# TensorE reads the present tile's slot and piece count at the top of the round instead of between y's transpositions and the second product

## The reference

```
# attention: y[b,h,t] = r_t (state + u k_t v_t); state = w_t * state + k_t v_t
x  = attention output as 3072 rows of 384
# first expert layer (float32)
expert_idx = argmax(normalised x @ normalised expert_emb.T / tau)
out[mask]  = gate_w[mask] * (relu(x[mask] @ w1[e]) @ w2[e])        # w1: 384x1024, w2: 1024x384
# second expert layer, on the rows of the first
e_idx = argmax(x @ w_gate)
out[mask] = gate_w[mask] * sigmoid(x @ w_output_gate)[e] * (relu(x[mask] @ w1[e]) @ w2[e])
```

## Time and profile before

| | |
|---|---|
| median of 3 runs | 810.31 us |
| the profiled execution | 813.64 us, its span from first to last instruction 811.9 us |
| granted TensorE clock, mean | 0.964 |
| PE busy | 727.1 us, 90% of the span |
| PEld (weight loads) busy | 638.3 us, 79% |
| DVE, ACT, POOL busy | 62%, 48%, 20% |

### The profile page before, as it was taken

The page is one execution under the profiler, slowest core; times in us unless marked ns, Lnnn a source line. Parts: engine busy times, 40 slices in busy tenths (PEclk is TensorE's granted clock), DMA queues, the critical chain, the costliest instruction groups (busy, mean ns, idle before and its releaser), DMA issues.

```text
span 811.9 us, 21320 instructions
## 1 busy us (share of the span) xinstructions
PE 727.1 (90%) x5494; PEld 638.3 (79%) x5495; DVE 503.7 (62%) x1363; ACT 390.8 (48%) x760; POOL 160.3 (20%) x202
## 2 busy tenths in 40 slices
PE   2898898980899999999999998499999999999994
PEld 2687687760688988888888887379999999999993
DVE  8899899986466674746675675544635444436621
ACT  4565777781355463535464464144534444425521
POOL 5354565553000000000000000001000000010000
PEclk9999999996799999999999999689999999999998
DMA  5655588635543351423352433233505152416110
GB/s 130 148 148 151 156 251 238 176 99 188 185 157 116 117 175 37 135 91 109 117 173 91 141 116 117 91 101 132 202 29 194 49 182 78 157 39 194 39 33 26
DMA packets 50267, 103.73 MB, mean 128 GB/s; under 512 B 7921, under 2 KB 29904, under 8 KB 50224
## 3 DMA queue, kind: packets, MB, share of 16 engines
q1 hardware_dynamic: 29536, 67.18, 26.9%
q10 hardware_dynamic: 15568, 21.76, 9.8%
q0 software_dynamic: 5120, 14.26, 4.8%
HBM read 85.73 MB, written 19.01 MB: 129 GB/s over the span
## 4 chain that ended last, share of the span: by engine, by line
PE 69%; DVE 8%; issue 8%; ACT 5%; DMA 4%; ACTq 2%; SPq 2%; POOL 1%; DVEq 0%; POOLq 0%
PE bank L1303 18%; PE bank L1329 17%; PE bank L1337 10%; PE bank L1308 9%; PE bank L1318 5%; DMA rk<-rk_in 3%; PE bank L1270 2%; PE bank L1292 2%; ACT wall L559 2%; DVE SF L765 2%; DVE Q L756 2%; PE bank L1124 1%; ACTq L246 1%; PE bank L1263 1%; POOL rkp L393 1%
## 5 line engine op out<-in xcount | busy, mean ns | idle before, releaser
L1303 PE MATMUL bank<-wall,xT_hi 128*128 (+1 forms) x660 | 180.1, 409 | 3.3 <-ACT xT_hi L651 3.3
L1329 PE MATMUL bank<-wall,hT_hi 128*128 x880 | 167.2, 341 | 0.8 <-ACT hT_hi L660 0.5
L1329 PEld LDWEIGHTS bank<-wall,hT_hi 128*128 128x128 f32 x880 | 154.6, 189 | 8.1 <-issue 5.5
L869 DVE TENSOR_TENSOR wall<-raw,wall 128x1024 f32 (+1 forms) x96 | 112.0, 1221 | 61.9 <-ACT wall L559 58.6
L1303 PEld LDWEIGHTS bank<-wall,xT_hi 128*128 128x128 f32 x660 | 119.7, 192 | 24.0 <-issue 4.0
L655 ACT ACTIVATE hs<-bank 128x512 f32<-128x512 f32 x110 | 65.1, 592 | 110.6 <-PE bank L1308 103.5
L559 ACT ACTIVATE wall<-raw 128x1024 f32 (+1 forms) x96 | 95.1, 1050 | 42.0 <-issue 42.0
L1308 PE MATMUL bank<-wall,xT_lo 128*128 (+1 forms) x330 | 94.5, 394 | 0.0
L660 ACT ACTIVATE hT_hi<-bank 128x512 fp32r<-128x512 f32 x110 | 59.8, 596 | 68.6 <-PE bank L1318 68.6
L1337 PE MATMUL bank<-wall,hT_lo 128*128 x440 | 91.0, 348 | 0.0
L1030 DVE TENSOR_TENSOR xT_lo<-bank,xT_hi 128x384 fp32r<-128x384 f32 x57 | 31.8, 558 | 87.9 <-ACT xT_hi L651 87.9
(11 more groups left out here) (194 smaller groups left out, 953.7 us busy)
## 6 DMA issues: line engine op xcount, KB each, us to landing
raw<-wall_in SPq DMA_DIRECT2D x96, 512.0 KB, 3.8
xin<-sorted ACTq DMA_DIRECT2D x59, 194.0 KB
rk<-rk_in SPq DMA_DIRECT2D x46, 192.0 KB
v_in<-v_src ACTq DMA_DIRECT2D x24, 192.0 KB
vT<-vT_in ACTq DMA_DIRECT2D x48, 96.0 KB
wb<-w_in SPq DMA_DIRECT2D x46, 96.0 KB
sorted<-padrow SPq DMA_DIRECT2D x16, 194.0 KB, 2.1
sorted<-yrow,slot POOLq DMA_INDIRECT x28, 2.6
```

What stands on the lines that cost most here:

```text
L869: v.tensor_tensor(w_lo[:, slot, cols], raw[:, q], w_hi[:, slot, cols].bitcast(F32), ALU.subtract).then_inc(w_split, 1)
L1303: pe.matmul(bank[n][:, :], xT_hi[:, k, :], w[:, bass.ds(slot, 1), cols].rearrange("p o n -> p (o n)"), start=(k == 0 and w is w_hi), stop= ...
L1329: pe.matmul(bank[2][:, 0:DM], hT_hi[:, j, :], w[:, bass.ds(slot, 1), W2 + j * DM:W2 + (j + 1) * DM].rearrange("p o n -> p (o n)"), start=( ...
```

## The change

The one line that loads the present tile's slot and piece count is moved up, behind the load of the next tile's.

```diff
@@ -1349,11 +1349,11 @@
                 with pe.Fori(0, last) as p:
                     slot, pieces = weights(p + 1)
+                    old_slot, old_pieces = weights(p)
                     transpose_h(p)
                     first_product(p + 1, 0, slot, pieces)
                     if m == 0:
                         transpose_y(p + 1)
-                    old_slot, old_pieces = weights(p)
                     second_product_hi(p, old_slot, old_pieces)
                     if m == 0:
                         logits_y(p + 1)
```

## The result

| | before | after |
|---|---|---|
| median of the runs | 810.71 us (6 runs, 808.7 to 811.85) | 851.67 us (6 runs, 849.94 to 854.34) |
| ratio | | 1.0508, 95% interval 1.0488 to 1.0528 |
| span of the profiled execution | 811.9 us | 852.6 us |
| granted clock, mean | 0.964 | 0.964 |

The kernel is 5% slower. It was forecast at 852.9 us, within 842 to 861.

What follows compares the result with a forecast made beforehand. TensorE (PE) was taken to bound both loops, with sequencer time free only while it is ahead. 25.5 + 9.6 - 2.0 + 9.5 = 42.6 us on a median of 810.31 gave 852.9 us, range 842 to 861.

Steps and rivals of the forecast that it cites:

- Cost of `weights`: Both loops: one `weights` call takes TensorE's sequencer 1.5 us, with bounds of 1.03 and 1.77 us.
- Slack in m=0: Top of m=0's rounds: sequencer's slack 0.43 us after rounds without splits, 0 after splits; VectorE's choice of expert sets it.
- Sum of m=0: Loop of m=0: 25.5 us at 17 tops without slack, plus 9.6 at nine others, less 2.0 in the middle.
- Middle: m=0, ahead of L1329: the 0.2 us wait goes, worth 2.0 us over 10 rounds without splits.
- Slack in m=1: Top of m=1's rounds: slack 1.15 us against 1.5 us added, costing 9.5 us over 27 rounds.
- C: Both loops: the sequencer reaches the top earlier by what the middle saves; 2.0 us faster, 808.3 us; chance 0.04.
- E: Both loops: the loads move but are done beside PE's work anyway; time within 0.2%; chance 0.03.
- Rival D: Loop of m=0: the clock falls to 0.96 as well, adding 5.6 us, time 858.5 us; chance 0.07.

Runs made afterwards that it cites:

- mid_early: The kernel before with the middle pair of loads moved one step earlier, ahead of `transpose_y`; 809.55 us, ratio 0.9975.
- carry: The kernel before with the present tile's two numbers copied in registers instead of loaded a second time; 808.98 us, ratio 0.9974.
- extra_top: The kernel before with an unused pair of value loads added at the top of each round, middle pair kept; 852.61 us, ratio 1.0489.
- only_m1: The kernel before with the read moved to the top in the loop of m=1 alone; 817.84 us, ratio 1.0072.
- extra_late: The kernel before with an unused pair of value loads added ahead of `ranks_y`, middle pair kept; 812.33 us, ratio 1.0017.

## Why the prediction was right, point by point

- **Cost of `weights`, 1.5 us.** Right. The wait is 1.57 to 1.70 us in the rounds after splits, 1.64 on the mean; 0.08 of it stood there before, and 0.04 comes back in the transpositions (below).
- **Slack in m=0 and its place.** Right. Waits of about 1.1 us after rounds without splits (1.5 - 0.43 = 1.07) and 1.6 after the others. The branch still follows VectorE's choice, by 0.10 to 0.14 us in all 26 rounds both before and after, and not the sequencer's saved time; in one round of the kernel after, L993 and the branch:

```profile
323.79 0.29 DVE L993 TENSOR_SCALAR oha<-iota,r 128x8 bf16<-128x8 f32 x1
```

```profile
L1350 PEldq ALU_OP  x1: 32/32/32, 324.2 to 324.2; - x1
```

- **Sum of m=0, forecast 33.1 us.** Measured 34.0: the first top comes 1.47 us later (within the trace, 3.95 us behind the value load of L1349 where it came 2.42); the round behind that entry is 1.50 longer; seven with the first pieces split 1.66 each; eight with the last split 1.51; ten without splits 0.74 on the mean (nine 0.86, and the last 0.36 shorter, since the transpositions behind the loop have no added pair ahead of them and the middle's wait is gone). The seven are 0.15 over the term of 1.5. The prediction had ScalarE's chain shift as a whole, but in these rounds it also grew: `yT` is used 7.14 us behind the first weight load of L1318 where it was 7.03. Behind its copies of `hT_hi` ScalarE does register work of its own before the splits, and one value load there (L246) takes 472 to 542 ns in the kernel after where it took 281 to 286. In the round of 290.31 ScalarE stands before the splits for 1.98 us, in the same round before for 1.74:

```profile
294.07 2.95 ACT L559 ACTIVATE wall<-raw 128x1024 f32 x3 [1.98 <-issue]
```

```profile
284.48 2.96 ACT L559 ACTIVATE wall<-raw 128x1024 f32 x3 [1.74 <-issue]
```

- **Middle, -2.0 us.** The size was right (`mid_early` 2.6 us less in the loop's trace, `carry` 1.9), the cause incomplete. The loads are indeed not done when PE has transposed y. But the prediction laid this on their own length and place: `extra_top` keeps them and has no wait, `mid_early` moves them past one step and has none. They are late because the pair begins behind the hold at L1263 and its second load then takes some 0.26 us longer than usual. The prediction had the 577 ns in its rows and used them only as an upper bound for the top, where no load is that long.
- **Slack in m=1, forecast 9.5 us.** The mis-sized term. The wait is 8.9 us in 26 rounds, 0.34 each, as forecast; a round grows by only 9.81 - 9.58 = 0.23, and the loop by 5.4 us in all (the first round is 0.2 and the last 0.1 us shorter). I had taken each missing 0.1 us of lead as 0.1 us of time. But L1318 to L1303 shrinks from 0.94 to 0.82: before, the first weight load of L1318 starts while L1337's last matmuls still run, and its own matmul starts 0.18 us behind it; after, it starts with PE idle, and its matmul 0.01 us behind it (medians of 27 rounds). So 0.12 us of each wait was time that the weight load would have spent waiting in any case. The same 0.12 us is in the rounds of m=0 behind a round without splits. That the running matmul is the reason is read from the order of the records; no run takes it by itself.
- **Rivals C and E.** Out: the kernel is 5% slower.
- **Rival D, the clock.** Out: 1.00 in the loop of m=0 with 36 us of waiting in it.
- **The total.** 34.0 for m=0, 5.4 for m=1 and 1.3 between the loops make the 40.7 by which the spans differ. The 1.3 us is not the change's: that stretch takes 32.2 to 34.2 us over all the kernels, and 1.2 us more than before in `only_m1`, `carry` and `mid_early` too. The place of the first top varies likewise (210.1 to 215.5 us), so the cost of 1.5 us there is better read from its distance to L1349. The forecast of 42.6 was 1.9 over the measured 40.7: +4.1 in m=1, -0.9 in m=0, -1.3 between the loops. That it came so near is in part luck: these errors take off from each other.

So what the same two loads cost went by the sequencer's lead where they stood. At the top of m=0 it had next to none in 16 of the 25 rounds behind the first (0.17 to 0.24 us from the last assertion to L1318), and the wait there was 1.6 us; in the nine others it had some 0.43, and the wait was 1.1. In m=1 it had 1.15, and a round grew by 0.23. Ahead of `ranks_y` the sequencer stood for 1.86 us in m=0 and 1.31 in m=1 (medians), the added pair took 1.24, and the kernel got no longer (ratio 1.0017).

## What to carry to other kernels

Read the sequencer's lead over its engine at each place where register work stands (last register instruction to the first instruction that needs it), and look for the holds that reset it. Here they were an instruction that waited for data (the pair's first load 0.16 us behind `ybuf`, the branch of m=0 0.10 to 0.14 behind `oha`), and in m=1 PE's backlog (16 weight loads to start at the branch). Ask what register work would cost just ahead of such a hold: here 1.24 us of it cost nothing in holds of 1.31 and 1.86 us, and the same pair at the top, behind them, 41 us. Don't count on time saved ahead of a hold: the pair taken out of the middle of m=0 left the branch as far behind `oha` as it was.

## What the runs showed of the hardware

- In the loops TensorE's sequencer took its register work (the value loads and address work of PEldq) in the order of the program, and ahead of PE: at the branch of m=1, 16 weight loads and 17 matmuls of the round that ends were still to start, in 27 of 27 rounds of the kernel before and of the one after.
- A wait of the weight loads was more than the loss: with matmuls of the same engine running up to it, 0.34 us of idle weight loading in m=1 cost 0.23 us of the round.
- An instruction of TensorE that waited for data held the sequencer too, so that not even register work for later instructions was done (`ybuf` ready at 304.69, the pair begun at 304.7; the pair's first load 0.16 us behind `ybuf` in 25 of 25 rounds).
- Some value loads took up to 587 ns where the median is 302, and the hold at L1263 by itself didn't stretch them (308 ns behind it in the last round of `extra_late`). In the loop of m=0, over all eleven traces, 131 value loads begin 2.57 to 2.76 us behind ScalarE's issue of the next tile's rows (`xin`, L647 in the kernel before), and 116 of them take more than 400 ns; of the 2785 others two do. They are TensorE's, ScalarE's and VectorE's. In the kernel before it is 23 of TensorE's, in the kernel after nine of ScalarE's and none of TensorE's. What in that time stretches them stays open.
- Copying two registers at both ends of the round cost nothing that shows in m=1, where the sequencer has a lead of 1.15 us: in `carry` its round is 9.58 us as before.
